# A two-layer MoE behind chunked linear attention: tiles of 512 tokens in place of 384

## The reference

```python
for t in range(S):                      # attention: a state of 48x48 for each head
    state = alpha[:, :, t, :, None] * state + einsum('bhd,bhe->bhde', k[:, :, t], v[:, :, t])
    y[:, :, t] = einsum('bhd,bhde->bhe', q[:, :, t], state)
x = y.transpose(0, 2, 1, 3).reshape(3072, 384)

h = x @ w_in                            # first layer, 384 -> 2048 -> 384
P = a[0] + a[1]*h + a[2]*h*h + a[3]*h*h*h
Q = 1.0 + abs(b[0])*abs(h) + abs(b[1])*h*h
x = (P / (Q + 1e-06)) @ w_out

h = x @ w_in2                           # second layer, 384 -> 1024 -> 384
e = exp(h - max(h)); solu = h * e / (sum(e) + 1e-09)
ln = (solu - mean(solu)) / sqrt(var(solu) + 1e-06) * g_ln
out = ln @ w_out2
```

## Time and profile before

| | us |
|---|---|
| median of the runs | 801.46 |
| profiled execution | 799.91 |
| its span, first to last instruction | 798.1 |
| TensorE busy | 773.5 (97%) |
| VectorE busy | 688.1 (86%) |
| ScalarE busy | 593.4 (74%) |
| GpSimd busy | 303.9 (38%) |

### The profile page before, as it was taken

One profiled execution on the slowest core, in us unless ns is written; L12 is line 12 of the kernel. 1 busy time (PEld: TensorE's weight loads), 2 busy tenths in 40 slices (PEclk: granted clock), 3 DMA queues, 4 the chain that ended last, 5 costly groups with the idle time before them and its releaser, 6 DMA issues.

```text
span 798.1 us, 16327 instructions
## 1 busy us (share of the span) xinstructions
PE 773.5 (97%) x5406; PEld 720.8 (90%) x5406; DVE 688.1 (86%) x1251; ACT 593.4 (74%) x1214; POOL 303.9 (38%) x405
## 2 busy tenths in 40 slices
PE   7999999799899999999999999999999999999998
PEld 6777778698799999999999999999999999999988
DVE  6999999799998898889888988898889888988854
ACT  6777778688877786778677867787778777877743
POOL 4999998122223232323232323232323232323211
PEclk9999999999999999999999999999999999999999
DMA  8999999200100010001000000000000000000000
GB/s 190 220 244 261 240 248 255 66 1 1 31 1 1 10 41 11 1 12 39 10 0 14 35 10 0 21 28 10 0 35 14 10 0 10 11 11 6 5 21 30
DMA packets 93542, 42.96 MB, mean 54 GB/s; under 512 B 80632, under 2 KB 90432, under 8 KB 93504
## 3 DMA queue, kind: packets, MB, share of 16 engines
q1 hardware_dynamic: 88944, 28.92, 15.2%
q0 software_dynamic: 4560, 13.57, 5.8%
HBM read 33.04 MB, written 9.44 MB: 53 GB/s over the span
## 4 chain that ended last, share of the span: by engine, by line
PE 68%; DVE 14%; ACT 9%; issue 4%; DMA 2%; SPq 1%; ACTq 0%; DVEq 0%; POOL 0%
PE h_ps L1172 18%; PE acc_ps L1198 18%; PE y_ps L1154 12%; PE z_ps L1216 12%; PE chunks_ring L337 2%; DVE work L1416 2%; PE z_ps L1226 2%; DVE rec L1408 2%; DVE den L1404 2%; DMA chunks_kin<-in_k_dram 2%; ACT rec L1305 1%; ACT g_hi L1295 1%; DVE chunks_kp L624 1%; DVE chunks_err L617 1%; DVE chunks_rec L620 1%
## 5 line engine op out<-in xcount | busy, mean ns | idle before, releaser
L1355 POOL TENSOR_TENSOR g_lo<-work,g_hi 128x384 fp32r<-128x384 f32 x128 | 130.8, 1022 | 401.5 <-ACT g_hi L1295 401.5
L1172 PE MATMUL h_ps<-x,w 128*128 (+1 forms) x1143 | 224.8, 340 | 6.0 <-DVE work L1426 4.4
L1198 PE MATMUL acc_ps<-g_hi,w 128*128 128x384 f32 x768 | 218.3, 338 | 2.3 <-POOL g_lo L1355 2.3
L1172 PEld LDWEIGHTS h_ps<-x,w 128*128 128x128 f32 x1143 | 200.5, 188 | 12.3 <-DVE work L1426 8.5
L1198 PEld LDWEIGHTS acc_ps<-g_hi,w 128*128 128x128 f32 x768 | 141.2, 188 | 2.8 <-POOL g_lo L1355 2.8
L1267 ACT ACTIVATE h<-h_ps 128x384 f32<-128x384 f32 x128 | 61.7, 482 | 98.9 <-PE h_ps L1172 98.8
L1198 PE MATMUL acc_ps<-g_lo,w 128*128 128x384 f32 x384 | 129.7, 338 | 0.0
L1421 DVE SCALAR_TENSOR_TENSOR den<-h,ncoef,den 128x384 f32<-128x384 f32 x128 | 78.6, 614 | 39.9 <-ACT den L1270 39.0
L1216 PE MATMUL z_ps<-w,x 128*128 128x512 f32 x396 | 99.9, 397 | 2.4 <-DVE lnT L1438 2.4
L1154 PE MATMUL y_ps<-w,lnT 128*128 128x384 f32 x528 | 99.9, 338 | 0.0
L1295 ACT ACTIVATE g_hi<-work 128x384 fp32r<-128x384 f32 x128 | 68.1, 532 | 38.2 <-DVE work L1416 35.0
(11 more groups left out here) (162 smaller groups left out, 1120.8 us busy)
## 6 DMA issues: line engine op xcount, KB each, us to landing
chunks_kin<-in_k_dram SPq DMA_DIRECT2D x32, 144.0 KB, 3.7
chunks_vin<-in_v_dram SPq DMA_DIRECT2D x16, 288.0 KB, 4.7
wstage<-in_moe_w_in_dram POOLq DMA_DIRECT2D x9, 512.0 KB, 5.0
attention_out<-solu SPq DMA_DIRECT2D x64, 72.0 KB, 3.1
out_dram<-ysb SPq DMA_DIRECT2D x24, 192.0 KB, 1.8
work<-in_alpha_dram SPq DMA_DIRECT2D x30, 144.0 KB, 4.3
chunks_qin<-in_q_dram POOLq DMA_DIRECT2D x28, 144.0 KB, 4.8
x<-attention_out SPq DMA_DIRECT2D x7, 576.0 KB, 3.9
```

Source lines behind the costliest of these rows:

```text
L1172: mm = nc.tensor.matmul(h_ps[:, s % 2, 0:TT], w1[:, wz, kc, s * P:(s + 1) * P], xs[:, xz, kc, :], start=(n == 0), stop=(n == 3 * KC - 1))
L1198: mm = nc.tensor.matmul(acc_ps[:, dc, 0:TT], w2[:, wz, f, dc * P:(dc + 1) * P], rhs, start=(f == 0 and n == 0), stop=(f == FC1 - 1 and n = ...
L1355: nc.gpsimd.tensor_tensor(g_lo[:, 1 - o, :], gate[:, 1 - o, :], g_hi[:, 1 - o, :].bitcast(F32), ALU.subtract).then_inc(glo_done, 1)
```

## The change

Tiles of 512 tokens, 6 of them, across the borders of the batches. The scratch in DRAM is one array of 384 rows by 3,072 tokens instead of eight of 384 by 384. `x` is one buffer (high and low), and raw tokens have a buffer `xraw` beside it, so the split is no longer in place; all of it is done in step 15, after the last h products of the tile before. `den` has one buffer; `h2` is gone, the square goes into `rec`, and Abs comes last of the three and waits for `rec_done` of the chunk before; `gate` is written over `num`; `shift` is written into `ysb`. VectorE's part of SPLIT stands ahead of `den`, `num1`, `num2` instead of behind them. A tile has 4 blocks, which start at steps 3, 7, 11 and 15, with schedules of their own for the last tile and the last but one. Masks and bounds of the attention live in `solu` and its mask product in a buffer of its own.

```diff
+def tokens_of(scratch, first, count):
+    return scratch.rearrange("(c p) t -> p c t", p=P)[:, :, bass.ds(first, count)]
 def first_tokens(sp, scratch, over):
+    sp.dma_start(over.raw, tokens_of(scratch, 0, over.raw.shape[2])).then_inc(over.x0_loaded, 16)
...
-                        scratch[bass.ds(m // PPB * 2 + z, 1), bass.ds(m % PPB * (2 * D) + j * D, D), :].rearrange("o d t -> (o d) t"),
+                        scratch[bass.ds(m % PPB * (2 * D) + j * D, D), bass.ds(m // PPB * S + z * HS, HS)],
...
                 act.wait_ge(ksq_seen, NPAIR)
+                act.wait_ge(k_turned, NPAIR)
...
-    TT = S // 2
-    NT = NB * 2
+    TT = 512
+    NT = NB * S // TT
...
-        STEPS = [[start + lag for lag in (0, 1, 1, 2, 2, 3, 3, 4, 4, 5, 6, 6, 7, 8)] for start in (3, 8, 13)]
+        STEPS = [[start + lag for lag in (0, 1, 1, 2, 2, 3, 3, 4, 4, 5, 6, 6, 7, 8)] for start in (3, 7, 11, 15)]
+        LAST_BUT_ONE_STEPS = STEPS[:2] + [[11, 12, 12, 13, 13, 14, 14, 15, 15, 16, 17, 17, 17, 18],
+                                            [15, 16, 15, 16, 16, 17, 17, 18, 18, 19, 19, 20, 20, 21]]
         LAST_STEPS = [[3, 3, 3, 3, 4, 5, 5, 6, 6, 6, 6, 7, 6, 8],
                       [4, 5, 4, 5, 5, 6, 6, 7, 7, 8, 7, 9, 7, 9],
-                      [6, 7, 6, 7, 7, 8, 7, 9, 9, 10, 8, 10, 8, 10]]
+                      [6, 7, 6, 7, 7, 8, 7, 9, 9, 9, 8, 10, 8, 10],
+                      [7, 8, 7, 8, 8, 9, 8, 10, 10, 11, 9, 11, 9, 11]]
...
 # SyncE
-                        wait_alone(sp, h_ready, i * FC1, carrier)
-                        wait_alone(sp, x_loaded, i * 16, carrier)
-                        load(i + 1, (i + 1) % 2)
+                        wait_alone(sp, x_ready, i * KC + KC, carrier)
+                        load(i + 1)
...
 # ScalarE
+                            act.wait_ge(y_stored, 16 * t + 16)
+                            nc.scalar.activation(ysb[:], means[:], ACT.Copy, scale=sm(NMG)).then_inc(shift_ready, 1)
...
                             act.wait_ge(h_ready, g + 1)
-                            if not (i_is(i, 0) and s == 0):
-                                act.wait_ge(den_ready, g)
-                            nc.scalar.activation(h2[:], hp, ACT.Square)
+                            if s == FC1 - 1 and (not isinstance(i, int) or i < NT - 1):
+                                for kc in range(KC):
+                                    x_hi(i + 1, kc)
                             if not (i_is(i, 0) and s < 2):
                                 act.wait_ge(g_done, g - 1)
-                            nc.scalar.activation(den[:, o, :], hp, ACT.Abs, scale=coef[:, 4:5]).then_inc(hw_ready, 1)
+                            nc.scalar.activation(rec[:, o, :], hp, ACT.Square)
+                            if not (i_is(i, 0) and s < 2):
+                                act.wait_ge(glo_done, g - 1)
                             nc.scalar.activation(num[:, o, :], hp, ACT.Identity, bias=ncoef[:, 2:3],
                                                  scale=ncoef[:, 3:4]).then_inc(num0_done, 1)
+                            if not (i_is(i, 0) and s == 0):
+                                act.wait_ge(rec_done, g)
+                            nc.scalar.activation(den[:], hp, ACT.Abs, scale=coef[:, 4:5]).then_inc(hw_ready, 1)
...
 # VectorE
                             dve.wait_ge(num2_done, gp + 1)
                             dve.wait_ge(rec_done, gp + 1)
-                            if not (i_is(i, 0) and s < 3):
-                                dve.wait_ge(glo_done, gp - 1)
-                            nc.vector.scalar_tensor_tensor(out=gate[:, p, :], in0=num[:, p, :], scalar=ncoef[:, 0:1], in1=rec[:, p, :],
+                            nc.vector.scalar_tensor_tensor(out=num[:, p, :], in0=num[:, p, :], scalar=ncoef[:, 0:1], in1=rec[:, p, :],
                                                            op0=ALU.add, op1=ALU.mult).then_inc(g_done, 1)
+                        if s == FC1 - 1 and (not isinstance(i, int) or i < NT - 1):
+                            for kc in range(KC):
+                                x_lo(i + 1, kc)
                         t = block_at(i, s, SPLIT)       # SPLIT as before, now followed by:
+                            nc.vector.scalar_tensor_tensor(out=den[:], in0=rec[:, o, :], scalar=ncoef[:, 5:6], in1=den[:],
+                                                           op0=ALU.mult, op1=ALU.add).then_inc(den_ready, 1)
...
-                            dve.wait_ge(y_stored, 16 * t + 16)
                             dve.wait_ge(shift_ready, t + 1)
-                            nc.vector.scalar_tensor_tensor(out=ysb[:], in0=y_of(i, s, OUT), scalar=sm(GAIN), in1=shift[:],
+                            nc.vector.scalar_tensor_tensor(out=ysb[:], in0=y_of(i, s, OUT), scalar=sm(GAIN), in1=ysb[:],
                                                            op0=ALU.mult, op1=ALU.add).then_inc(ysb_ready, 1)
```

More of the change, by code:

```diff
@@ L55 @@
 class Handover:
-    work: object
+    raw: object
     x: object
@@ L134, in attention_by_chunks @@
         att_stored, y_copied, x0_loaded = over.att_stored, over.y_copied, over.x0_loaded
-        qin, kin, rec, att, causal, seen, okay, ext = homes
-        ain = over.work.rearrange("p a b t -> p (a b t)")[:, 0:2 * NC * ROWS].rearrange("p (o c d) -> p o c d", o=2, c=NC)
+        qin, kin, rec = homes
+        ain = over.raw.rearrange("p c t -> p (c t)")[:, 0:2 * NC * ROWS].rearrange("p (o c d) -> p o c d", o=2, c=NC)
+        att = sb("att", [P, 2, NC, P])
         vin = sb("vin", [P, 2, 2, NC, D])
@@ L522, in body @@
                 act.wait_ge(ksq_seen, NPAIR)
-                for kc in range(over.x.shape[3]):
-                    nc.scalar.activation(over.x[:, 0, HI, kc, :], x0_of(over.work, *over.x.shape[3:])[:, kc, :],
-                                         ACT.Copy).then_inc(over.xhi_done, 1)
+                act.wait_ge(k_turned, NPAIR)
+                for kc in range(over.x.shape[2]):
+                    nc.scalar.activation(over.x[:, HI, kc, :], over.raw[:, kc, :], ACT.Copy).then_inc(over.xhi_done, 1)
             act.wait_ge(y_done, n)
@@ L590, in body @@
                 dve.wait_ge(kp_ready, NPAIR)
-                for kc in range(over.x.shape[3]):
+                for kc in range(over.x.shape[2]):
                     dve.wait_ge(over.xhi_done, kc + 1)
-                    nc.vector.tensor_tensor(over.x[:, 0, LO, kc, :], x0_of(over.work, *over.x.shape[3:])[:, kc, :],
-                                            over.x[:, 0, HI, kc, :].bitcast(F32), ALU.subtract).then_inc(over.x_ready, 1)
+                    nc.vector.tensor_tensor(over.x[:, LO, kc, :], over.raw[:, kc, :],
+                                            over.x[:, HI, kc, :].bitcast(F32), ALU.subtract).then_inc(over.x_ready, 1)
             wait(dve, y_done, m)
@@ L677, in attention_by_scan @@
         qT, kT, aT, vT = xT
-        masked = over.work.rearrange("p a b t -> p (a b t)")[:, 0:S]
+        masked = over.raw.rearrange("p c t -> p (c t)")[:, 0:S]
         kv = sb("kv", [P, S])
@@ L815, in vector @@
             dve.wait_ge(over.h_ready, 1)
[L816 to L818 removed]
+            for kc in range(over.x.shape[2]):
+                tokens = over.raw[:, kc, :]
+                nc.vector.tensor_copy(over.x[:, HI, kc, :], tokens).then_inc(x_again, 1)
                 dve.wait_ge(x_again, 2 * kc + 1)
[L820 removed]
+                nc.vector.tensor_tensor(over.x[:, LO, kc, :], tokens, over.x[:, HI, kc, :].bitcast(F32),
                                         ALU.subtract).then_inc(x_again, 1)
[L822 removed]
+            dve.wait_ge(x_again, 2 * over.x.shape[2])
         dve.sem_inc(joined, 1)
@@ L964, in build @@
         lnT = sb("lnT", [P, 2, FC2, P], F32R)
-        h2 = sb("h2", [P, TT])
-        den = sb("den", [P, 2, TT])
-        num, gate = work[:, 0], work[:, 1]
+        den = sb("den", [P, TT])
+        num = sb("num", [P, 2, TT])
         rec = sb("rec", [P, 2, TT])
@@ L1048, in block_in @@
                     continue
-                for j, steps in enumerate(LAST_STEPS if i_is(tile, NT - 1) else STEPS):
+                for j, steps in enumerate(steps_of(tile)):
                     if steps[stage] == s + FC1 * rounds:
@@ L1068, in y_of @@
         def y_of(i, s, stage):
-            return acc_ps[:, 2, 0:DM] if last_block(i, s, stage) == 1 else y_ps[:, 0:DM]
+            return acc_ps[:, 2, 0:DM] if last_block(i, s, stage) in (1, 3) else y_ps[:, 0:DM]
         def solu_of(i, s, stage):
-            return work[:].rearrange("p a b t -> p (a b t)")[:, 0:F2] if last_block(i, s, stage) == 1 else solu[:]
+            return num[:].rearrange("p a t -> p (a t)") if last_block(i, s, stage) in (1, 3) else solu[:]
         def lnT_of(i, s, stage):
             j = last_block(i, s, stage)
-            if j in (1, 2):
-                return x[:, j - 1].rearrange("p z c t -> p (z c t)")[:, 0:2 * F2].rearrange("p (z f t) -> p z f t", z=2, f=FC2)
+            if j in (1, 2, 3):
```

(3 more changed lines are left out.)

105 lines of the change are left out of this document (45 added, 60 removed).

## The result

The changed kernel takes 804.6 us (median of 15 runs, 801.84 to 807.85) against 801.38 (15 runs, 799.88 to 802.55) for the kernel before on the same chip: ratio 1.0041, interval [1.0026, 1.0056]. It is slower by 0.4%. The profiled execution took 803.01 us (span 801.3) against 799.91 (798.1).

What follows compares the result with a forecast made beforehand. TensorE was taken to bound the long steady part and last blocks, VectorE tile 0. Terms -1.8 - 1.3 + 0.8 + 3.1 + 0.9 = +1.7 us on the 801.46 us median gave 803.2 us, 80% range 796.5 to 810.

Steps and rivals of the forecast that it cites:

- The sign: Whole kernel: forecast slower, +1.7 us; chances given were slower 0.47, same 0.24, faster 0.29.
- Term 1: TensorE's product groups: 191 of 512 columns at 2.10 us replace 255 of 384 at 1.58; -1.8 us (-5.6 to +0.1).
- term 3: Steady part: old lnT waits go, step 15 gains a wait (+5.4), small gaps shrink; +0.8 us (-5 to +4).
- Term 5: Attention's end: longer x_hi/x_lo and first h products, raw tokens maybe later; +0.9 us (+0.3 to +2).
- Rival A: All 191 groups: 512-column h and acc products run faster, 2.06 us a group; price 7.6 us, 795.6 us; chance 0.17.
- Term 2: Tile 0, where VectorE sets the pace: steps of 4.4 us, TensorE idle 9.5 instead of 10.8; -1.3 us (-3 to +4).
- the ring of `den`: Tile 0: Abs waits for the previous chunk's rec, a circle over VectorE and ScalarE of together 4.4 us.
- rival C: Tile 0: each hop of den's circle costs 0.1 more, 4.7 us a step; step 19's cover gone; 811 us; chance 0.20.
- the forecast's 4.0 and 0.6: Steady part: six waits of z for lnT vanish (-4.0 us), remaining small gaps shrink with fewer groups (-0.6 us).
- rival B: Step 15: TensorE's wait for lnT is covered, so -5.4 us, 797.8 us; chance 0.12.
- Term 4: Last blocks: y of block 3 waits for OUT to free y_ps, solu turn +0.4; +3.1 us (0 to +5).

Runs made afterwards that it cites:

- experiment 1: Changed kernel with VectorE's lnT subtraction moved ahead of the three x_lo in step 15: 798.65 us, ratio 0.9967 to the kernel before.
- Experiment 2: Changed kernel with VectorE's OUT moved ahead of lnT and x2 in step 2 of the last round: 801.62 us, ratio 1.0006 to the kernel before.
- experiment 8: Kernel before (384 tokens) with only the attention's output scratch changed to one array: 801.92 us, ratio 0.9998.
- experiment 7: Changed kernel (512 tokens) with VectorE's lnT subtraction put back behind num2: 890.26 us, ratio 1.111 to the kernel before.
- experiment 10: Changed kernel with both VectorE moves (experiment 1, Experiment 2), 30 filling TensorE products around tile 0, and Abs ahead of Identity for the first chunk: 794.47 us, ratio 0.9922.
- experiment 5: Kernel before (384 tokens) with only VectorE's lnT subtraction moved ahead of den, num1 and num2: 802.66 us, ratio 1.0011.
- experiment 3: Changed kernel with 30 unused products of 512 columns filling TensorE's idle time around tile 0: 802.88 us, ratio 1.0023 to the kernel before.
- experiment 4: Kernel before (384 tokens) with one den buffer, the square in rec, and Abs last, waiting for the previous chunk's rec: 813.51 us, ratio 1.0146.

## Why the prediction was right

The sign stands, and each of the five terms came out within its stated range. The size is a weaker success: +3.2 us in the medians for +1.7, nearly twice, with misses of -1.0, +1.5 and +1.0 in terms 1, 3 and 5 that partly cancel. What term 3 had wrong is two steps of TensorE in round 1.

**Term 1, the pace: -1.8 forecast.** Groups start 2.09 and 2.10 us apart, products 232.8 ns on average. 191 groups at 2.095 are 400.1 us, against 402.9: -2.8. Rival A (2.06) is out. So is the Trainium skill's "TensorE: Matmul & The Clock Gate" (back-to-back issue gap) with 131 ns for load and product pairs at 512 columns: these pairs, at full clock, are 233 ns apart.

**Term 2, tile 0: -1.3.** From the second h group (152.17) to the first acc of tile 1 (237.87) it is 85.70 us and was 68.82, +16.88. The work in it grew by 18.0 (35 groups at 2.095 for 55.3), so idle time by -1.1. The parts cancelled: the step is 4.32 us and not 4.4, -1.4 over 17 steps. It is VectorE's six instructions back to back (4.35 in the forecast); the ring of `den` was not the longer of the two, so rival C's 4.7 is out. The start and the turn into tile 1 are longer by about as much.

**Term 3, the steady part: +0.8.** As forecast, the waits at step 7 are gone in rounds 2 to 4 and step 15 has one in rounds 1 to 4: 1.32, 1.40, 1.40 and 1.40 us by the starts (1.35 forecast). Not forecast: in round 1 step 7 waits too, 1.38 us. The forecast gave TensorE "6.3 or 7.15 us in each step". In steps 5 and 6 these times need the y products of the fourth block of the tile before (G4A and G4B come six and seven steps behind a block's start; in the code SHIFT stands between them), and in round 1 there is no such block: h groups start at 248.39, 252.56 and 257.54, so the steps take 4.17 and 4.98 us, against 6.29 and 7.18 one round later, where these stand in them:

```profile
355.39 2.28 PE L1157 MATMUL y_ps<-w,lnT 128*128 128x384 f32 x12
...
362.50 2.34 PE L1157 MATMUL y_ps<-w,lnT 128*128 128x384 f32 x12
```

VectorE is not late from tile 0, which was the forecast's condition ("they would stay if VectorE still ran a step late"). In step 5 it waits for Abs in round 1 as in round 2:

```profile
252.56 0.75 DVE L1435 SCALAR_TENSOR_TENSOR den<-rec,ncoef,den 128x512 f32<-128x512 f32 x1 [0.84 <-ACT den L1278]
...
355.38 0.75 DVE L1435 SCALAR_TENSOR_TENSOR den<-rec,ncoef,den 128x512 f32<-128x512 f32 x1 [0.83 <-ACT den L1278]
```

From 252.56 on it works without a pause until the subtraction of lnT at 262.45, and TensorE, through with its two short steps, waits for that. This is read from the trace; no run tests it. So term 3 is +2.3 for +0.8 (6.9 of new waits, less the forecast's 4.0 and 0.6). For the four waits of step 15 experiment 1 shows the cause (1.51 us a round from the order of VectorE's program alone), and with it that rival B had no cover.

**Term 4, the last blocks: +3.1.** y waits once, 2.55 us by the starts (2.7 forecast), and the two turns 0.36 and 0.35: 3.2. Experiment 2 takes 2.57 away.

**Term 5, the attention's end: +0.9.** The second h group comes 1.89 us later. 0.37 of it is the longer x_lo and 0.52 the longer h group, as forecast; 1.0 is there before either, in the attention. My suspects were the raw tokens and the stores, and experiment 8 clears the layout. The profiles of the other kernels, all with the same attention, point to its own DMAs. This is TensorE's wait for k in the changed kernel and in experiment 7's:

```profile
PE chunks_turn_k L331 <- DMA chunks_kin<-in_k_dram: 2.2, 3, 0.8
```

```profile
PE chunks_turn_k L331 <- DMA chunks_kin<-in_k_dram: 0.5, 1, 0.5
```

With 0.5 us of it the first h group starts at 143.84, with 0.6 (experiment 10) at 143.81, with 2.0, 2.2 and 2.4 at 144.44, 144.66 and 144.98; the kernel before had 0.5 and 143.29. So at equal waits about 0.5 us is left, near the 0.37 forecast. The waits do not settle it alone: experiment 2's profile has 0.3 and starts at 144.25, and at 384 tokens experiment 5's has 1.5 and starts at 146.38, later than any at 512. Most of the 1.0 varies from execution to execution. Whether such waits are more frequent at 512 tokens (1.3 to 2.4 us in four of seven profiles, and 1.1 and 1.5 in two of five at 384) is open.

**The sum.** -2.8 - 1.1 + 2.3 + 3.2 + 1.9 = +3.5 by the measured sizes; the last product ends 3.18 us later (798.27 for 795.09; the 0.6 for small gaps in term 3 is the forecast's figure and was not measured apart). The forecast had +1.7. The difference is term 5 (+1.0) and round 1's wait (+1.4), less a microsecond of pace.

**The clock**, which the forecast left at 1.00. The +3.1 us of the profiled executions has nothing of it, as the stretch at the lower level costs nothing in tile 0. How much of the +3.2 of the medians is clock is not shown: at a mean clock of 1.000 the changed kernel has one execution, of 801.84 us, and experiment 3 has five of 802.0 to 802.85, against about 800.1 for the kernel before, so some +1.7 to +2.4 are there without it. The kernel before loses clock as well (mean clocks of 0.995 to 1.000 in its runs). The profile of experiment 8, at 384 tokens, shows it behind acc's wait of 2.26 us at 219.34 (window; busy times; granted clock 0.54):

```profile
219.34:223.00 3.66, 3.66 (x12) 3.48 (x13) 3.49 (x8) 1.79 (x5) 0.00 (x0) 0.54 0.01 2
```

Here TensorE sets the pace, and round 1 takes 78.93 us, where the profile of the kernel before, at 1.00 in this place, has 77.40. The same loss that is free in tile 0 at 512 tokens costs 1.5 us.

**What a right number hid.** Rival C had `den` matter in tile 0 alone, since "from tile 1 on TensorE's step is 6.3". That is so only where the products of a block fill each step. In experiment 4 TensorE has steps of 3.2 us between the blocks, and 9 of the 12 us lie in the rounds, which I had expected unchanged. The forecast took the even spacing into its number and did not name it as the condition on which the shared `den` is cheap. Experiment 7 is the other half: the early lnT subtraction, which I had priced at the 4.0 us of the old waits, holds off 86 us here. At 384 tokens the same edit is worth nothing (experiment 5).
